# A retention layer and two MLPs in one kernel: which engine prepares the operands of the first span, of the fourth product and of the second layer

## The chip, the cores and the metric

The kernel runs on one core of one Trainium2 chip. TensorE (PE) multiplies, VectorE (DVE), ScalarE (ACT) and GpSimd (POOL) prepare and finish its operands, and SyncE (SP) issues every DMA. The metric is the time of one execution on the device in microseconds; the median of three runs is quoted. Lower is better.

## The reference

```python
gamma = 1.0 - 2.0 ** (-5.0 - np.arange(8))
for t in range(768):                         # retention, batch 4, 8 heads of 64
    state = gamma * state + einsum('bhd,bhe->bhde', k[:, :, t], v[:, :, t])
    y[:, :, t] = einsum('bhd,bhde->bhe', q[:, :, t], state) / 8
x = y.transpose(0, 2, 1, 3).reshape(3072, 512)
h = x @ w_in;  x = (h * cos(h)) @ w_out      # layer 1, 512 -> 2048 -> 512
h = x @ w_in2                                # layer 2, the same sizes
g = where(h >= 1, h, where(h <= -1, 0, (h + 1) ** 2 / 4))
return g @ w_out2
```

All arrays are float32.

## The kernel before

**Retention.** The 768 steps are cut into 6 chunks of 128, and the heads into 4 pairs, which gives 24 units. A unit has four input tiles of 128x512: q and k by columns, k and v by rows. q is multiplied by a table of decays (`scale_q`), k by rows by another (`scale_k`). PE makes `scores(u)` from k and q; DVE writes them, masked, to SBUF (`mask`); PE makes `outputs(u)` from v, the masked scores and the state of its head pair; PE makes `outer(u)`, which is added to the state (`update_state`).

**The two layers.** Each layer's first product, x times the up weights, is done with seven products p1 to p7 of half size instead of eight (a Strassen form), so that sums of quarters of x and of the weights are needed: s3, s2 and s1 are the sums behind p7, p6 and p5, and a fourth, s4 = x12 - s2, is the operand of p3. Every operand goes to PE as a pair of reduced-precision parts: ACT copies the number to the high part (`split_high` to `x_hi`, `t_high` to `tw`, `wd_high` to `wd_hi`, `gate_high` to `g_hi`), and then the low part is the number minus the high part (`split_low` and `gate_low` on DVE, `t_low` and `wd_low` on POOL). A product is then three matmuls for each of two contraction tiles, so six in all, of 128x512 output (L489, L491, L493); a down product (`down`, L518 to L524) is twelve.

**The order.** There are six spans, each of 2 chunks (1024 rows): three for layer 1 and three for layer 2. A span has 8 quads. Quad q > 0 is p1, p6, a down product, p2, p7, p5, a down product, p4, p3. After the quads a tail of 18 down products runs; in it, between the down products, the units of the next span are worked (spans 1 and 2), or the x of the next span comes back from DRAM (`x2_scratch`) and is summed and split (before spans 3, 4 and 5). Each engine's order is written out by hand in its own loop, and engines meet only at semaphores: an engine that waits holds back all that is behind it in its loop.

**The prologue** (L530 to L544 on PE, L784 to L794 on DVE, L992 to L1000 on ACT, L1099 to L1113 on POOL) works the 8 units of span 0. DVE scales q of units 0 and 1, POOL scales q of units 2 to 7 and k of all 8, and at unit 4 sums the first quad's up weights (`t_sums(0)`, `t_sums(1)`); `t_low(0)` and `t_low(1)` stand before the q of unit 7 and after it:

```python
for u in range(AHEAD):          # POOL, L1105
    if u >= 2:
        scale_q(u)
    scale_k(u)
    if u == 4:
        t_sums(0)
        t_sums(1)
    if u in (6, 7):
        t_low(u - 6)
```

As the loop shows, `t_low(0)` follows unit 6 and so precedes `scale_q(7)`. PE's p1 and p7 of quad 0 (`EARLY_PRODUCTS`) stand between `outer(6)` and `outputs(7)`. The weights of quad 1 are split by ACT and POOL inside quad 0.

**The queues.** SP's one queue issues every load in the order of the sync block. The up weights of a quad land in one half of a ring of two (`raw`, `tw`); in the spans 0 and 3 (`made(s)`) they are summed and split there and stored to `t_scratch`, in the others they are read back from it. The down weights of a layer are split once. Layer 1's are split one pair per quad of span 0 (`wd_high(0, q)`, `wd_low(0, q)`). Layer 2's are split in the tail of span 2 for q = 0 to 5 (L1029, L1136) and in the first two quads of span 3 for q = 6 and 7 (L976, L1124). The sums of x for layer 2 are eight POOL instructions per span (`x2_sum_s3`, `x2_sums_rest`, L1079); those of layer 1 are eight DVE instructions per span (`x_sum`: L643, and L629 for s4), and all fourteen low parts of x are DVE's (L653 from PSUM, L656 from SBUF).

Of the kernel before, what the change touches and what calls it, by code (L numbers as in the profile page):

```python
# [7 lines left out]
F32 = mybir.dt.float32  # L8
# [32 lines left out]
EARLY_PRODUCTS, LATER_PRODUCTS = ["p1", "p7"], ["p2", "p6", "p5", "p4", "p3"]  # L41
# [9 lines left out]
SPLITS = [("p1", 0, X11), ("p1", 1, X11 + 1), ("p2", 0, X12), ("p2", 1, X12 + 1), ("p7", 0, X11), ("p7", 1, X11 + 1),  # L51
          ("p4", 0, X22), ("p6", 0, SUM2), ("p5", 0, X21), ("p3", 0, X12),
          ("p4", 1, X22 + 1), ("p6", 1, SUM2 + 1), ("p5", 1, X21 + 1), ("p3", 1, X12 + 1)]
NS = len(SPLITS)
SUMS_BEFORE = {4: 1, 5: 2, 7: 3, 8: 4, 9: 5, 11: 6, 12: 7, 13: 8}
NSUM = 8
# [17 lines left out]
SPLITS_LATE = [[0], [1], [2], [3], [4], [5], [6], [7], [8, 9], [10, 11], [12, 13], []]  # L74

SPLITS_OF = [[0], [1], [2], [3], [4], [5], [6, 7, 8, 9], [10, 11, 12, 13]]
# [15 lines left out]
def retention_mlp_kernel(nc, q_t, k_t, k_n, v_n, w1u, w1d, w2u, w2d, table, out):  # L92
# [7 lines left out]
    with ExitStack() as ctx:  # L100
# [17 lines left out]
        tb = sb("tb", [P, TABLE_WIDTH])  # L118
        half_one = sb("half_one", [P, 1])
        probe = sb("probe", [P, 1])  # L120

# [12 lines left out]
        kn_sb = nc.alloc_sbuf_tensor_at("kn_sb", [P, N], F32, offset=place + 8 * N * 4)  # L134

# [74 lines left out]
        q_scaled_first, q_scaled, kn_scaled = sem("q_scaled_first"), sem("q_scaled"), sem("kn_scaled")  # L210
        scores_done, masked = sem("scores_done"), sem("masked")
        y_done, outer_done, state_done = sem("y_done"), sem("outer_done"), sem("state_done")
        x_copied = sem("x_copied")
        x2_summed = sem("x2_summed")
        x2_in = [sem(f"x2_in{i}") for i in range(8)]
        summed, xhi_done, xlo_done = sem("summed"), sem("xhi_done"), sem("xlo_done")
        raw_in = [[sem(f"raw_in{i}_{kt}") for kt in range(2)] for i in range(2)]
# [153 lines left out]
        def _(pe):  # L371
            def y_taken(u):
# [3 lines left out]
                if i < KT:  # L376
                    pe.wait_ge(xlo_done, NS * s + i + 1)
                elif i < COPIES:
                    pe.wait_ge(summed, NSUM * s + i - KT + 1)
                else:  # L380
                    pe.wait_ge(xlo_done, NS * s + (7 if i == COPIES else 11))
                    pe.wait_ge(summed, NSUM * s + (4 if i == COPIES else 7))

# [23 lines left out]
            def outputs(u):  # L407
# [12 lines left out]
                if has_state:  # L420
                    pe.wait_ge(state_done, 2 * (u - KT + 1))
# [12 lines left out]
            def outer(u):  # L434
# [3 lines left out]
                pe.wait_ge(kn_scaled, u + 1)  # L438
                if u < AHEAD:
                    if u >= 2:  # L440
# [731 lines left out]
```

## Time and profile before

| what | value |
|---|---|
| median of 3 runs | 1144.98 us |
| lowest, highest | 1143.63, 1147.88 us |
| the profiled execution: its time | 1146.63 us |
| the profiled execution: its span | 1144.8 us |
| PE busy in the span | 1104.1 us, 96% |
| DVE, ACT, POOL busy | 709.8, 506.3, 261.6 us |

The span is what the profiler saw from the first to the last instruction; the execution's own time is 1.8 us more. Busy time of PE counts overlapping matmuls, so a busy share near 1 does not say at which pace they start: the number of matmuls in a stretch does. The page names a line of the kernel for every group, and the tile that is written before the arrow, the tiles that are read behind it.

### The profile page before, as it was taken

How to read it: one execution, taken by the hardware profiler on the slowest of the kernel's cores; microseconds unless marked ns; L12 is line 12 of the kernel's file. 1: busy time of each engine (PE TensorE's matmuls, PEld its weight loads, DVE VectorE, ACT ScalarE, POOL GpSimd, SP SyncE). 2: the span in 40 equal slices, each digit the busy share in tenths (PEclk: the TensorE clock that was granted, in tenths of full speed). 3: DMA queues.
4: the chain of work that ended last, by engine and by line, in shares of the span. 5: the costliest groups of instructions: out<-in, count | busy, mean ns of one | idle time of the engine just before them, and what ended most of it. 6: DMA issues, size and time to landing. Idle time of an engine off the chain costs nothing.

```text
span 1144.8 us, 14409 instructions
## 1 busy us (share of the span) xinstructions
PE 1104.1 (96%) x5572; PEld 893.7 (78%) x5572; DVE 709.8 (62%) x1016; ACT 506.3 (44%) x822; POOL 261.6 (23%) x251
## 2 busy tenths in 40 slices
PE   7789999989999999999997999999999999999998
PEld 6667777877888787788875788887888887888887
DVE  5677775474666646466659677656566647566642
ACT  2367764234656423565654343434322334333232
POOL 6366652320000120000118565504000004000000
PEclk8899999999999999999999999999999999999999
DMA  9234553442333243233233633343233331233111
GB/s 342 102 121 183 202 208 124 148 138 110 129 129 126 105 139 120 101 129 129 83 104 118 237 116 141 159 171 133 101 129 129 116 114 74 102 129 129 65 38 37
DMA packets 44452, 149.12 MB, mean 130 GB/s; under 512 B 4704, under 2 KB 4832, under 8 KB 42336
## 3 DMA queue, kind: packets, MB, share of 16 engines
q1 hardware_dynamic: 44384, 148.20, 36.1%
q8 instruction: 44, 0.72, 0.3%
q14 instruction: 24, 0.20, 0.1%
HBM read 106.24 MB, written 41.94 MB: 129 GB/s over the span
## 4 chain that ended last, share of the span: by engine, by line
PE 69%; DVE 12%; ACT 8%; POOL 3%; DMA 3%; issue 3%; SPq 1%; DVEq 0%; ACTq 0%
PE bank L489 11%; PE bank L493 10%; PE bank L491 10%; PE bank L522 7%; PE bank L524 7%; PE bank L523 7%; PE bank L518 5%; PE bank L519 4%; PE bank L520 4%; DVE g_lo L714 4%; ACT work L927 2%; DVE x_lo L656 2%; ACT work L929 2%; PE bank L402 2%; DMA kn_sb<-in_k_n 2%
## 5 line engine op out<-in xcount | busy, mean ns | idle before, releaser
L489 PE MATMUL bank<-x_hi,tw 128*128 128x512 f32 x672 | 269.0, 400 | 9.7 <-ACT work L900 4.1
L491 PE MATMUL bank<-x_lo,tw 128*128 128x512 f32 x672 | 266.9, 397 | 0.0
L493 PE MATMUL bank<-x_hi,tw 128*128 128x512 f32 x672 | 266.8, 397 | 0.0
L518 PE MATMUL bank<-g_hi,wd_hi 128*128 128x512 f32 x384 | 154.2, 402 | 11.7 <-DVE g_lo L714 10.9
L489 PEld LDWEIGHTS bank<-x_hi,tw 128*128 128x128 f32 x672 | 127.5, 190 | 44.8 <-DVE late L705 4.0
L493 PEld LDWEIGHTS bank<-x_hi,tw 128*128 128x128 f32 x672 | 127.6, 190 | 30.3
L522 PE MATMUL bank<-wd_hi,g_hi 128*128 128x512 f32 x384 | 150.3, 391 | 0.8 <-DVE g_lo L714 0.8
L519 PE MATMUL bank<-g_lo,wd_hi 128*128 128x512 f32 x384 | 150.7, 392 | 0.0
L520 PE MATMUL bank<-g_hi,wd_lo 128*128 128x512 f32 x384 | 150.5, 392 | 0.0
L491 PEld LDWEIGHTS bank<-x_lo,tw 128*128 128x128 f32 x672 | 127.7, 190 | 29.1
L524 PE MATMUL bank<-wd_hi,g_lo 128*128 128x512 f32 x384 | 149.8, 390 | 0.0
L523 PE MATMUL bank<-wd_lo,g_hi 128*128 128x512 f32 x384 | 149.6, 389 | 0.0
L714 DVE SCALAR_TENSOR_TENSOR g_lo<-late,g_hi 128x512 fp32r<-128x512 f32 x96 | 85.2, 887 | 90.0 <-ACT g_hi L943 89.6
L943 ACT ACTIVATE g_hi<-late 128x512 fp32r<-128x512 f32 x96 | 60.3, 630 | 151.0 <-PE bank L520 80.5
L714 DVE SCALAR_TENSOR_TENSOR g_lo<-work,g_hi 128x512 fp32r<-128x512 f32 x96 | 85.7, 892 | 42.6 <-ACT g_hi L943 40.6
L931 ACT ACTIVATE work<-work,half_one 128x512 f32<-128x512 f32 x96 | 66.9, 720 | 94.3 <-DVE work L694 94.3
L943 ACT ACTIVATE g_hi<-work 128x512 fp32r<-128x512 f32 x96 | 60.7, 632 | 92.3 <-DVE work L708 54.7
L518 PEld LDWEIGHTS bank<-g_hi,wd_hi 128*128 128x128 f32 x384 | 72.4, 188 | 34.5 <-DVE g_lo L714 17.0
L1079 POOL TENSOR_TENSOR work<-work 128x512 f32<-128x512 f32 x24 | 37.4, 1586 | 219.1 <-DVE x_lo L656 219.1
L522 PEld LDWEIGHTS bank<-wd_hi,g_hi 128*128 128x128 f32 x384 | 72.1, 188 | 18.0 <-DVE g_lo L714 2.9
L520 PEld LDWEIGHTS bank<-g_hi,wd_lo 128*128 128x128 f32 x384 | 72.5, 189 | 15.9
L524 PEld LDWEIGHTS bank<-wd_hi,g_lo 128*128 128x128 f32 x384 | 72.1, 188 | 15.4
(91 smaller groups left out, 1467.8 us busy)
## 6 DMA issues: line engine op xcount, KB each, us to landing
tw<-t_scratch SPq DMA_DIRECT2D x64, 896.0 KB, 6.3
t_scratch<-tw SPq DMA_DIRECT2D x16, 1792.0 KB, 7.8
work<-x_scratch SPq DMA_DIRECT2D x24, 256.0 KB, 3.7
raw<-in_w1u SPq DMA_DIRECT2D x16, 256.0 KB, 3.1
wd_raw<-in_w1d SPq DMA_DIRECT2D x8, 512.0 KB, 8.9
q_sb<-in_q_t SPq DMA_DIRECT2D x16, 256.0 KB, 2.9
k_sb<-in_k_t SPq DMA_DIRECT2D x16, 256.0 KB, 3.8
v_sb<-in_v_n SPq DMA_DIRECT2D x16, 256.0 KB, 4.1
```

The lines of the kernel that those rows point to most:

```text
L489: nc.tensor.matmul(to[:, :], w[:, kt, 0, i, :], x_hi[:, i, kt, :], start=opens, stop=False, skip_group_check=True)
L491: nc.tensor.matmul(to[:, :], w[:, kt, 0, i, :], x_lo[:, i, kt, :], start=False, stop=False, skip_group_check=True)
L493: last = nc.tensor.matmul(to[:, :], w[:, kt, 1, i, :], x_hi[:, i, kt, :], start=False, stop=kt == 1, skip_group_check=True)
L518: nc.tensor.matmul(to[i][:, :], wd_hi[:, f, cols], g_hi[:, slot, :], start=opens, stop=False)
L519: nc.tensor.matmul(to[i][:, :], wd_hi[:, f, cols], g_lo[:, slot, :], start=False, stop=False)
L520: last = nc.tensor.matmul(to[i][:, :], wd_lo[:, f, cols], g_hi[:, slot, :], start=False, stop=closes)
L522: nc.tensor.matmul(to[i][:, :], g_hi[:, slot, cols], wd_hi[:, f, :], start=opens, stop=False)
L523: nc.tensor.matmul(to[i][:, :], g_hi[:, slot, cols], wd_lo[:, f, :], start=False, stop=False)
L524: last = nc.tensor.matmul(to[i][:, :], g_lo[:, slot, cols], wd_hi[:, f, :], start=False, stop=closes)
L714: nc.vector.scalar_tensor_tensor(out=g_lo[:, d % 2, :], in0=g, scalar=2.0 if s < PAIRS else 1.0, in1=g_hi[:, d % 2, :].bitcast(F32), op0=A ...
L931: nc.scalar.activation(t, t, ACT.Square, scale=0.5, bias=half_one[:, 0:1]).then_inc(square_done, 1)
L943: nc.scalar.activation(g_hi[:, d % 2, :], g, ACT.Copy, scale=2.0 if s < PAIRS else 1.0).then_inc(ghi_done, 1)
```

## The change

**Prologue.** The k of the first 8 units is scaled by ACT (`scale_k` there, two instructions of 256 columns per unit) and no longer by POOL. The first state of each head pair (units 0 to 3) is copied from PSUM by ACT (`copy_state`) and not by DVE. POOL does q of units 2 to 5, the sums of quad 0's weights, q of 6 and 7, then the low parts of quad 0's weights, the sums and low parts of quad 1's, whose high parts ACT does in the prologue too. PE's p1 and p7 move behind the last unit, and quad 0's order is p1, p7, p2, p6, p5, p4, p3. DVE masks two units ahead.

**The operand of p3.** In spans 0, 1 and 2 the sum s4 and its low part move from DVE to POOL (`x3_operand`), four instructions per span; the high part stays with ACT, at the end of its list. In all spans `sum_u3` and `sum_h22` of quad 0 now wait for these low parts.

**Layer 2.** The eight sums of x per span move from POOL to DVE (`x2_sum`), and the high and low parts stand in another order, spread over the tail (`SUMS_LATE`, `HIGHS_LATE`, `LOWS_LATE`). All eight pairs of the second layer's down weights are split within the quads of span 3.

**Addresses.** The tables `tb`, `half_one` and `probe` (656 + 1 + 1 columns) are allocated behind the weight ring and no longer ahead of it, so the ring lies lower in each partition.

```diff
-EARLY_PRODUCTS, LATER_PRODUCTS = ["p1", "p7"], ["p2", "p6", "p5", "p4", "p3"]
+FIRST_OF_ALL = ["p1", "p7", "p2", "p6", "p5", "p4", "p3"]
+SUMS_LATE = {3: [("s3", 0), ("s3", 1)], 4: [("s2", 0), ("s1", 0)], 5: [("s4", 0)], 6: [("s2", 1), ("s1", 1)], 7: [("s4", 1)]}
+HIGHS_LATE = {0: [("p1", 0), ("p1", 1)], 1: [("p2", 0), ("p2", 1)], 4: [("p7", 0), ("p7", 1)], 5: [("p4", 0), ("p6", 0)],
+              6: [("p5", 0), ("p3", 0)], 7: [("p4", 1), ("p6", 1)], 8: [("p5", 1), ("p3", 1)]}
+LOWS_LATE = {1: [("p1", 0), ("p1", 1)], 2: [("p2", 0), ("p2", 1)], 4: [("p7", 0)], 5: [("p7", 1), ("p4", 0)], 6: [("p6", 0)],
+             7: [("p5", 0), ("p3", 0)], 8: [("p6", 1)], 9: [("p5", 1), ("p4", 1), ("p3", 1)]}
@@ PE
-            for u in range(AHEAD):
+            for u in range(AHEAD - 2):
                 outputs(u)
-                if u + 2 < AHEAD:
-                    scores(u + 2)
+                scores(u + 2)
                 outer(u)
-                if u == AHEAD - 2:
-                    pe.wait_ge(masked, 2 * (AHEAD - 1))
-                    for name in EARLY_PRODUCTS:
-                        product(0, 0, name)
+            outputs(AHEAD - 2)
+            outputs(AHEAD - 1)
+            outer(AHEAD - 2)
+            outer(AHEAD - 1)
@@ DVE
             def operands(s, i, lows=()):
...
+                    x_sum(s, "s2", kt)
+                    x_sum(s, "s1", kt)
+                    if s == 0:
+                        update_state(AHEAD - 2)
+                    split_low(s, "p6", kt)
+                    if lows:
+                        gate_low(s - 1, *lows.pop(0))
+                    split_low(s, "p5", kt)
+                    split_low(s, "p4", kt)
+                    for item in lows:
+                        gate_low(s - 1, *item)
@@ sum_u3, and in the same way sum_h22 with 2 * (s + 1)
                 if q == 0:
                     dve.wait_ge(u2_done, n + 1)
+                    dve.wait_ge(x3lo_done, 2 * s + 1)
@@ DVE, prologue
+            scale_q(1)
             mask(0)
-            scale_q(1)
-            dve.wait_ge(zeroed, KT)
+            mask(1)
             for u in range(AHEAD):
-                if u + 1 < AHEAD:
-                    mask(u + 1)
-                update_state(u)
                 operands(0, u)
+                if u + 2 < AHEAD:
+                    mask(u + 2)
+                if KT <= u < AHEAD - 2:
+                    update_state(u)
+            update_state(AHEAD - 1)
@@ DVE, tail before a span of layer 2
-                        if s + 1 < SPANS and n:
-                            for m in SPLITS_LATE[n - 1]:
-                                split_low(s + 1, m)
+                        if s + 1 < SPANS:
+                            for which, kt in SUMS_LATE.get(n, []):
+                                x2_sum(s + 1, which, kt)
+                            for name, kt in LOWS_LATE.get(n, []):
+                                split_low(s + 1, name, kt)
@@ ACT
-                if s == PAIRS and q in (0, 1):
-                    wd_high(1, QUADS - 2 + q)
-                more = n < QUADS * SPANS and made(n // QUADS)
+                more = 1 < n < QUADS * SPANS and made(n // QUADS)
...
-                if s == 0:
-                    wd_high(0, q)
+                if made(s):
+                    wd_high(s // PAIRS, q)
...
+            for u in range(3):
+                scale_k(u)
             for u in range(AHEAD):
                 operands(0, u)
-                if u == 4:
-                    t_high(0)
-                    t_high(1)
-                if u == AHEAD - 2:
-                    copy_p1(0, 0)
+                if u + 3 < AHEAD:
+                    scale_k(u + 3)
+                if u < KT:
+                    copy_state(u)
+                if u in (3, 4, 5):
+                    t_high(u - 3)
+                if u == 6:
+                    t_high(3)
@@ POOL
+            def x3_operand(s, kt):
+                x = work[:, X12 + kt, :]
+                pool.wait_ge(x_copied, COPIES * s + 2 + kt + 1)
+                pool.wait_ge(summed, NSUM * s + SUM_PLACE["s2", kt] + 1)
+                nc.gpsimd.tensor_tensor(x, x, work[:, SUM2 + kt, :], ALU.subtract).then_inc(x3_summed, 1)
+                pool.wait_ge(x3hi_done, 2 * s + kt + 1)
+                nc.gpsimd.tensor_tensor(x_lo[:, BLOCK["p3"], kt, :], x, x_hi[:, BLOCK["p3"], kt, :].bitcast(F32),
+                                        ALU.subtract).then_inc(x3lo_done, 1)
...
+            for u in range(2, 6):
+                scale_q(u)
+            t_sums(0)
+            t_sums(1)
+            scale_q(6)
+            scale_q(7)
+            t_low(0)
+            t_low(1)
+            t_sums(2)
+            t_sums(3)
+            t_low(2)
+            t_low(3)
+            x3_operand(0, 0)
+            x3_operand(0, 1)
             for s in range(SPANS):
                 for q in range(QUADS):
...
-                    if s == 0:
-                        wd_low(0, q)
-                    if s == PAIRS and q in (0, 1):
-                        wd_low(1, QUADS - 2 + q)
+                    if made(s):
+                        wd_low(s // PAIRS, q)
                 if s < PAIRS - 1:
...
+                    x3_operand(s + 1, 0)
+                    x3_operand(s + 1, 1)
```

## Rows read from the trace of the kernel before

**Rows 1.** The page, part 1: PE's line of the span.

```profile
PE 1104.1 (96%) x5572; PEld 893.7 (78%) x5572; DVE 709.8 (62%) x1016; ACT 506.3 (44%) x822; POOL 261.6 (23%) x251
```

**Rows 2.** Windows: stretch, length, busy time and count of each engine, granted clock, DMA.

```profile
40.00:60.00 20.00, 16.99 (x122) 13.57 (x119) 16.46 (x28) 8.23 (x14) 6.04 (x10) 0.81 0.33 119
60.00:80.00 20.00, 16.33 (x62) 12.24 (x62) 14.43 (x17) 13.27 (x22) 12.01 (x12) 0.91 0.42 145
...
603.00:640.40 37.40, 31.19 (x125) 23.82 (x125) 33.80 (x22) 16.15 (x25) 28.94 (x14) 0.95 0.26 85
...
80.00:184.00 104.00, 101.70 (x433) 80.48 (x431) 75.91 (x102) 74.31 (x119) 62.32 (x60) 1.00 0.54 191
...
300.00:380.00 80.00, 80.00 (x348) 65.23 (x347) 51.88 (x79) 47.77 (x79) 0.00 (x0) 1.00 0.31 115
660.00:760.00 100.00, 100.00 (x435) 81.48 (x434) 70.19 (x101) 41.40 (x60) 47.80 (x53) 1.00 0.41 155
780.00:800.00 20.00, 19.61 (x85) 15.42 (x84) 15.12 (x15) 8.76 (x16) 11.02 (x7) 1.00 0.17 67
```

**Rows 3.** Timeline of PE: start, length, line, tiles, count, idle before and its releaser.

```profile
24.93 1.16 PE L402 MATMUL bank<-first_in 64*128 64x128 f32 x16 [1.43 <-POOL first_in L1040]
...
37.20 2.00 PE L402 MATMUL bank<-late 64*128 64x128 f32 x16 [4.55 <-POOL late L1040]
...
43.00 0.50 PE L489 MATMUL bank<-x_hi,tw 128*128 128x512 f32 x1
...
45.89 1.05 PE L425 MATMUL bank<-late,state 128*128 128x128 f32 x8
...
47.80 0.64 PE L446 MATMUL bank<-late 128*64 128x64 f32 x16
...
63.44 0.50 PE L489 MATMUL bank<-x_hi,tw 128*128 128x512 f32 x1 [1.12 <-POOL tw L1068]
...
71.34 0.71 PE L489 MATMUL bank<-x_hi,tw 128*128 128x512 f32 x1 [2.08 <-ACT work L900]
...
255.96 0.50 PE L518 MATMUL bank<-g_hi,wd_hi 128*128 128x512 f32 x1 [1.12 <-DVE g_lo L714]
```

**Rows 4.** Timeline of POOL in the prologue and in quad 0.

```profile
23.52 1.27 POOL L1040 TENSOR_TENSOR first_in<-first_in,tb 128x512 f32<-128x512 f32 x1
...
35.79 1.26 POOL L1040 TENSOR_TENSOR late<-late,tb 128x512 f32<-128x512 f32 x1
...
61.28 2.10 POOL L1068 TENSOR_TENSOR tw<-raw,tw 128x896 fp32r<-128x896 f32 x1 [2.53 <-ACT tw L877]
```

**Rows 5.** The load of the last q: its issue on SP's queue, and its microseconds to landing.

```profile
16.93 0.36 SPq L247 DMA_DIRECT2D late<-in_q_t  x1
...
late<-in_q_t SPq DMA_DIRECT2D x1, 256.0 KB, 10.0
```

**Rows 6.** Timelines of DVE and of POOL in the tail of span 2.

```profile
602.53 0.68 DVE L656 TENSOR_TENSOR x_lo<-work,x_hi 128x512 fp32r<-128x512 f32 x1
...
606.23 1.78 DVE L656 TENSOR_TENSOR x_lo<-work,x_hi 128x512 fp32r<-128x512 f32 x1
...
622.01 2.88 DVE L656 TENSOR_TENSOR x_lo<-work,x_hi 128x512 fp32r<-128x512 f32 x1
...
603.21 12.74 POOL L1079 TENSOR_TENSOR work<-work 128x512 f32<-128x512 f32 x8 [25.20 <-DVE x_lo L656]
615.92 11.19 POOL L1075 TENSOR_TENSOR wd_lo<-wd_raw,wd_hi 128x1024 fp32r<-128x1024 f32 x4
```

**Rows 7.** Groups by line and shape: count, then busy time and mean ns of one.

```profile
L491 PE MATMUL bank<-x_lo,tw 128*128 128x512 f32 x672 | 266.9, 397 | 0.0
L519 PE MATMUL bank<-g_lo,wd_hi 128*128 128x512 f32 x384 | 150.7, 392 | 0.0
...
L877 ACT ACTIVATE tw<-raw 128x896 fp32r<-128x896 f32 x32 | 29.9, 939 | 1.5 <-POOL raw L1063 1.5
...
L1051 POOL TENSOR_TENSOR late<-late,tb 128x512 f32<-128x512 f32 x4 | 4.2, 1040 | 7.0 <-DMA late<-in_k_n 6.9
```

More of the change, by code:

```diff
@@ L456, in product @@
                 if q == 0:
-                    pe.wait_ge(xlo_done, NS * s + max(m for m in range(NS) if SPLITS[m][0] == name) + 1)
+                    if name == "p3":
+                        pe.wait_ge(x3lo_done, 2 * (s + 1))
+                    else:
+                        pe.wait_ge(xlo_done, NS * s + LOW_PLACE[name, 1] + 1)
                     if name in ("p7", "p4"):
@@ new lines, in split_low @@
+            def split_low(s, name, kt):
+                hi = x_hi[:, BLOCK[name], kt, :].bitcast(F32)
+                lo = x_lo[:, BLOCK[name], kt, :]
+                if name == "p3":
+                    dve.wait_ge(x3hi_done, 2 * s + kt + 1)
+                    nc.vector.tensor_tensor(lo, work[:, X12 + kt, :], hi, ALU.subtract).then_inc(x3lo_done, 1)
+                    return
+                slot = HIGHS[HIGH_PLACE[name, kt]][2]
+                dve.wait_ge(xhi_done, NS * s + HIGH_PLACE[name, kt] + 1)
+                if s < PAIRS and name not in SUM_OF:
+                    if name != "p4":
+                        dve.wait_ge(x_copied, COPIES * s + slot + 1)
+                    nc.vector.scalar_tensor_tensor(out=lo, in0=unit_banks(AHEAD * s + slot)[2][:, :], scalar=SCALE, in1=hi,
+                                                   op0=ALU.mult, op1=ALU.subtract).then_inc(xlo_done, 1)
@@ L840, in copy_x, with split_high @@
                 nc.scalar.activation(work[:, i, :], unit_banks(u)[2][:, :], ACT.Copy, scale=SCALE).then_inc(x_copied, 1)
-            def split_high(s, m):
-                name, kt, slot = SPLITS[m]
-                if s < PAIRS and m not in SUMS_BEFORE:
+            def split_high(s, name, kt):
+                hi = x_hi[:, BLOCK[name], kt, :]
+                if name == "p3":
+                    act.wait_ge(x3_summed, 2 * s + kt + 1)
+                    nc.scalar.activation(hi, work[:, X12 + kt, :], ACT.Copy).then_inc(x3hi_done, 1)
+                    return
+                slot = HIGHS[HIGH_PLACE[name, kt]][2]
+                if s < PAIRS and name not in SUM_OF:
@@ new lines, in scale_k, with copy_state @@
+            def scale_k(u):
+                p = u % KT
+                act.wait_ge(kn_in_first[u], 16)
+                for h in range(2):
+                    part = unit_kn(u)[:, :, h, :]
+                    last = nc.scalar.activation(part, part, ACT.Copy, scale=decay_k[:, 2 * p + h:2 * p + h + 1])
+                last.then_inc(kn_scaled_first, 1)
+            def copy_state(u):
+                act.wait_ge(outer_done, u + 1)
+                act.wait_ge(zeroed, u + 1)
+                for h in range(2):
+                    part = slice(h * DH, (h + 1) * DH)
+                    nc.scalar.activation(state[part, u, :, part],
+                                         unit_banks(u)[3][part, 0:B * DH].rearrange("p (b e) -> p b e", b=B),
+                                         ACT.Copy).then_inc(state_copied, 1)
@@ L1116, in _ @@
                     n = QUADS * s + q + 1
[L1117 removed]
+                    if 1 < n < QUADS * SPANS and made(n // QUADS):
                         t_sums(weight_item(n, 0))
```

237 lines of the change are left out of this document (103 added, 134 removed).

## The prediction, made before the kernel was changed

> **What bounds the kernel now.** I read the shares of the span first [rows 1]: PE is busy for 1104 of 1145 us, so an edit to ACT, DVE or POOL pays only where PE stands still or loses its clock. The windows [rows 2] show where. At its best pace PE starts 348 matmuls in 80 us (4.35 per us, 0.23 us each), in a window where POOL does nothing. Against that pace: 603 to 640.4 has 125, which 28.7 us would hold, so 8.7 us are lost; 80 to 184 has 433 in 104 us, so 4.5 us are lost; 780 to 800 has 85 in 20 us, 0.5 us lost; 660 to 760 loses nothing although POOL is busy for half of it. From 40 to 80 us the granted clock is 0.81 and 0.91, and PE idles for 7 us. The change touches all of these but 300 to 380, so each part is costed where PE stood.
>
> The timelines say why. In the tail of span 2 the same low part on DVE takes 0.68 us alone, 1.78 beside POOL's sums and 2.88 beside POOL's `wd_low` [rows 6]: the two engines take turns, each instruction waiting out the other's. In the prologue PE waits 4.55 us at 37.20 for the q of unit 7, which POOL scales at 35.79, behind `t_low(0)`, although it had landed at 16.93 + 10.0 = 26.9 us [rows 3 to 5]. Quad 1 starts at 63.44, held by `t_low` of its own weights, which POOL begins at 61.28 and which waited for ACT [rows 3, 4].
>
> **Part 1, prologue up to unit 7.** POOL's order is now q5, the sums of quad 0, q6, q7, with no k at all. The wait at 24.93 for q5 (1.43 us) shrinks, since q5 stands ahead of the sums: I take 0.9 of it. q7 no longer waits for `t_low(0)`: landed at 26.9, behind sums and q6, it is scaled at about 29 us, before PE can use it, so the 4.55 us go whole. Scores of unit 7 then start at 37.20 - 4.55 - 0.9 = 31.75. From there PE's own work to the first product is what it was: 5.8 us from 37.20 to 43.00, and 2.55 us for `outputs(7)` and `outer(7)` (45.89 to 47.80 + 0.64 [rows 3]); before `outputs(7)` I add 1 us for its mask, which stands behind s3's two instructions and POOL's turns on DVE. First product: 41 us, with all eight units done; before, this was 50.5.
>
> Who pays for that: ACT has 16 more instructions for k and 8 for the state. No row has this shape on ACT. Above, an instruction of 896 columns takes 0.94 us [rows 7], so 256 columns cost no more; below, nothing. I take 0.4 us each, by its share of the columns plus a fixed part, so 0.8 for a unit's k where POOL took 1.04 [rows 7]. They fall in ACT's gaps between units (ACT waits for PE's outputs), so I cost them at nothing; at 0.94 each, ACT would run 24 x 0.54 = 13 us more, half of it under the loads, and y of the last units would come some 4 us later.
>
> **Part 2, quad 0 and the start of quad 1.** p1, p7, p2, p6, p5 run from 41 to 48 (five times 6 x 0.23 = 1.4 us). Then p4 needs `sum_u3`, and p3 needs `sum_h22`; both now wait for p3's operand. Its chain starts when POOL has finished quad 1's `t_low(3)`, which I place at 43.1: the high part on ACT stands behind that of p5 for unit 6 and ends at 41.0, and POOL adds 2.1 [rows 4]. From 43.1: sum 1.3 (as a q on POOL [rows 4]), one turn of DVE 0.7, high part 0.6 (512 columns, by the 0.94 of 896 [rows 7]), low part 1.3, second sum 1.3, high part 0.6, low part 1.3, `sum_h22` 0.7: 7.8 us, so p3 can start at 51 and ends at 52.4. The weights of quad 1 have been ready since 43, so quad 1 starts at 52.4 and not 63.44: 11 us gained. Inside quad 1 the first down product needs `wd_low(0, 0)`, which cannot be earlier than its high part (at 53.5, behind quad 0's gate) and 1.1 for that high part and 2.8 on POOL (11.19 / 4 [rows 6]): 57.3, a stall of 2 us where PE had 0.5. But the p2 behind it was held at 71.34 by ACT's copy of p1, and its new date, by the same chain of down product, gates and sums without POOL's turns, is 60.3: still 11 us. I assume one fall of the clock to 1.2 GHz behind that stall, as there was one at 71.34 (0.71 us for a matmul there, 0.50 at 63.44). **Sum: -11.0 us**, from -14 (no x3 chain on the path) to -5 (ACT at 0.94 us, POOL waiting a turn at every step).
>
> **Part 3, spans 1 and 2.** DVE loses four instructions of 0.68 us at each transition, of which three stood ahead of the late `gate_low` that holds PE for 1.12 us at 255.96 [rows 3]. The order is shorter by one instruction there, so I take 0.6 us at this transition and 0.4 at the next. POOL's four instructions fall beside eleven microseconds of down products. **-1.0**, from -2 to +2 (POOL's turns delaying the last gates, or `sum_u3` waiting).
>
> **Part 4, tail of span 2 and the next two.** POOL has nothing left there. DVE has a down product's gate and at most three sums or low parts per down product: 4 x 0.61 = 2.44 us, against 12 x 0.23 = 2.76 us of PE. Each sum's inputs stand one down product or more ahead in the three lists, so that no engine waits in order. SP's order is unchanged, and the x tiles had landed when POOL used them at 603.21 [rows 6], before DVE will. So the whole loss goes: **-8.7** in span 2, **-0.5** in each of the two others, -9.7 in all; from -10.5 to -6.
>
> **Part 5, down weights in the quads of span 3.** Six more `wd_high` and `wd_low` there, one per quad. The model is span 0, which loses 4.5 us in 104 with POOL at 60%; but its DVE and ACT carry the cosine. Layer 2's window of 660 to 760 loses nothing with POOL at 48%, and `wd_low` would bring it to some 60%. I take +0.5, between 0 and +4.5, nearer the second because it is the same gate code.
>
> **Part 6, addresses.** A product's matmul takes 397 ns and a down product's 392 [rows 7], both 128x512. No row shows why. The ring's address may have a part in it or none: bounds 5 ns x 2016 matmuls, 10 us either way; I take 0, because no row ties a duration to a place.
>
> **Sum.** -11.0 - 1.0 - 9.7 + 0.5 = -21.2 us. The profiled execution took 1146.63 us, 1.65 above the median of 1144.98; its span of 1144.8 would become 1123.6 and its time 1125.4. Against the median: **1123.8 us**.
>
> **A rule against the change.** DVE does these two-input instructions in 0.68 us, and POOL takes 1.3 for a tile of the same size [rows 4, 6]: the operand of p3 moves to the slower engine and stands on the path in quad 0. The Trainium skill, "GPSIMD Engine Reference", section 4.1, says the same, that elementwise work with two inputs belongs on VectorE because GpSimd is about twice as slow; with the rows' durations for DVE the four steps would cost 2.4 us less in part 2. The skill's "SBUF — State Buffer", Terms, has the two engines share one pair of ports by a lock held for the whole instruction; the trace agrees by 1.78 and 2.88 against 0.68 us, and no estimate above needs the rule.
>
> **The rivals.**
> 1. *p3's operand takes over the wait in the prologue.* ACT and DVE wait in order for POOL (`turns` of quad 0 stands behind ACT's last high part of p3), so each turn lost on POOL moves everything. For it: POOL's chain has no slack in part 2. Against it: POOL's other work ends at 43. With 7 us more the time is 1131.
> 2. *The second layer's weights cost what the first's do.* +4 us more: 1128. For it: span 0; against it: the calm window of layer 2.
> 3. *The sums on DVE wait for the loads.* If the x tiles land after DVE asks, DVE holds the gates behind it and PE stops as before: half of part 4 comes back, 1128.5. Against it: POOL found them landed.
> 4. *The ring's new place makes product matmuls shorter* by up to 5 ns: 1114.
> 5. *Slower than before: the new place makes them longer.* Every product reads its weights from the ring. It decides from 21.2 us / 2016 = 10.5 ns per matmul on; at 14 ns the time is 1152. For it: the products are the slower kind already. Against it: the difference seen between two places and kinds is 5 ns.
>
> **How the numbers follow.** Forecast 0.66 (its own range 1118 to 1128), rival 1 0.13, rival 2 0.08, rival 3 0.04, rival 4 0.07, rival 5 0.02. The range of 8 in 10 takes in rivals 1 to 3 whole and a part of the fourth: 1116 to 1132. A measurement of this kernel tells 0.5%, 5.7 us, from no change. All cases but the fifth lie below 1139, so faster 0.95; rivals 1 and 3 together could end within it: same 0.03; slower 0.02.
>
> **What would show it.** Right: the first p1 of quad 0 near 41 us, p3 of it near 51, quad 1 near 52 to 53; PE's idle time before `down` on `gate_low` gone between 580 and 660; DVE's low parts of layer 2 at 0.69 us each in the tails and POOL idle there; some 88 matmuls per 20 us in span 3's quads. Wrong: a wait on `x3lo_done` over 3 us, on scores for a k scaled late by ACT, or on `wd_low` in span 3, or another mean for L491 than 397 ns.

## The result, and the profile after

The changed kernel takes **1113.65 us** (median of 4 runs, 1112.70 to 1114.66); the kernel before took 1145.99 in the 4 runs beside it (1143.63 to 1147.88). The ratio is 0.972 [0.970, 0.974]: 32 us less. The forecast was 1123.8, and the range ended at 1116.0, 2.4 us above the result. The profiled execution took 1114.66 us, its span is 1112.9.

The page of the changed kernel, its first line and its shares of the span, as [rows 1]:

```profile
span 1112.9 us, 14425 instructions
PE 1082.4 (97%) x5572; PEld 888.3 (80%) x5572; DVE 682.1 (61%) x1020; ACT 515.9 (46%) x846; POOL 232.9 (21%) x231
```

PE's busy time fell by 21.7 us (from 1104.1) with the same 5572 matmuls. An edit that only took stalls away would leave busy time as it was, unless the clock changed too. So either matmuls ran at a higher clock or something else happened; the next view shows both. (Two kernels below part the 21.7 us: with the ring back in its old place PE's busy time is 1094.4, so 9.7 go with the schedule and 12.0 with the ring.) Windows: the window, its length, busy time with instructions of PE, PE's weight loads, DVE, ACT and POOL, the granted clock, the DMA share and GB/s, as [rows 2]:

```profile
40.00:60.00 20.00, 17.31 (x79) 12.71 (x75) 16.22 (x24) 11.49 (x20) 13.55 (x14) 1.00 0.40 142
60.00:80.00 20.00, 18.18 (x78) 14.31 (x78) 13.31 (x20) 14.86 (x24) 11.30 (x13) 1.00 0.47 174
290.00:360.00 70.00, 70.00 (x311) 57.95 (x310) 46.39 (x71) 42.38 (x71) 0.00 (x0) 1.00 0.36 132
570.00:616.00 46.00, 45.61 (x201) 37.45 (x201) 25.06 (x40) 19.85 (x35) 0.00 (x0) 1.00 0.46 149
620.00:640.00 20.00, 17.86 (x71) 14.07 (x70) 16.32 (x21) 10.52 (x15) 17.29 (x21) 0.91 0.67 271
640.00:740.00 100.00, 100.00 (x442) 82.78 (x442) 71.38 (x101) 45.65 (x65) 61.48 (x58) 1.00 0.43 159
```

Three things stand here. The tail of span 2 (570 to 616) is full: 201 matmuls in 46 us, 4.37 per us, where [rows 2] have 125 in 37.4. The clock is at full speed from 40 to 80 us, where it was 0.81 and 0.91. And the calm window of 290 to 360 has 4.44 per us, *more than the 4.35 that the prediction called PE's best pace*. Nothing in the calm stretch waits, before or after. The matmuls themselves start sooner after each other. The lines of the product and of the down product, as [rows 7] (line, matmul, tiles and shape; busy us, mean ns of one; idle before):

```profile
L510 PE MATMUL bank<-x_lo,tw 128*128 128x512 f32 x672 | 262.2, 390 | 0.0
L538 PE MATMUL bank<-g_lo,wd_hi 128*128 128x512 f32 x384 | 150.1, 391 | 0.0
```

The product's matmul was 397 ns and is 390, the down product's was 392 and is 391. These durations overlap, so they give a sign and not a size. The size is the mean time from one matmul's start to the next, worked out from all the trace's matmuls inside a product or a down product: 232.7 ns before and 227.0 after in products, 227.7 and 227.3 in down products. 2016 product matmuls x 5.7 ns = 11.5 us.

**Where the 32 us lie.** I set each span's first product, and each tail's first down product, of one trace against the other's (us):

| stretch | gained |
|---|---|
| start to the tail of span 0 | 12.1 |
| transitions into spans 1 and 2 | -0.7, +0.2 |
| quads of spans 1 and 2 | 1.9, 1.9 |
| transition into span 3 | 9.3 |
| quads of span 3 | 0.4 |
| transitions into spans 4 and 5 | 1.1, 1.1 |
| quads of spans 4 and 5, last tail | 2.3, 2.3, 0.0 |

The quads of a span hold 336 product matmuls, so 5.7 ns each makes 1.9 us: the quads of spans 1 and 2 gain that by the pace alone. Those of spans 4 and 5 gain 2.3, and that is the ring's as well: in `ring_back` below they gain 0.0. The prologue's timeline (start, duration, engine, line, operation, tiles, and in brackets the wait and its releaser), as [rows 3], with one row from span 3 at its end:

```profile
31.59 1.16 PE L417 MATMUL bank<-late 64*128 64x128 f32 x16
37.18 1.13 PE L440 MATMUL bank<-late,state 128*128 128x128 f32 x8 [1.70 <-DVE late L618]
40.19 0.50 PE L508 MATMUL bank<-x_hi,tw 128*128 128x512 f32 x1
50.81 0.47 PE L508 MATMUL bank<-x_hi,tw 128*128 128x512 f32 x1 [0.64 <-DVE work L779]
52.27 0.39 PE L508 MATMUL bank<-x_hi,tw 128*128 128x512 f32 x1
56.41 0.47 PE L537 MATMUL bank<-g_hi,wd_hi 128*128 128x512 f32 x1 [1.26 <-issue]
59.25 0.49 PE L508 MATMUL bank<-x_hi,tw 128*128 128x512 f32 x1
628.39 0.79 PE L508 MATMUL bank<-x_hi,tw 128*128 128x512 f32 x1 [1.47 <-POOL tw L1137]
```

Scores of unit 7 at 31.59 (forecast 31.75), the first product at 40.19 (41), p3 of quad 0 at 50.81 (51), quad 1 at 52.27 (52.4), its first down product at 56.41 (57.3), its p2 at 59.25 (60.3). POOL's line, as [rows 4], shows p3's operand being made; both its low parts stand behind ACT for 0.74 us:

```profile
42.96 1.28 POOL L1151 TENSOR_TENSOR work<-work 128x512 f32<-128x512 f32 x1
44.98 1.57 POOL L1153 TENSOR_TENSOR x_lo<-work,x_hi 128x512 fp32r<-128x512 f32 x1 [0.74 <-ACT x_hi L892]
46.52 1.29 POOL L1151 TENSOR_TENSOR work<-work 128x512 f32<-128x512 f32 x1
48.55 1.29 POOL L1153 TENSOR_TENSOR x_lo<-work,x_hi 128x512 fp32r<-128x512 f32 x1 [0.74 <-ACT x_hi L892]
```

And DVE in the tail of span 2, as [rows 6]: the low part takes 0.69 us where it took up to 2.88 beside POOL.

```profile
592.08 0.69 DVE L753 SCALAR_TENSOR_TENSOR g_lo<-late,g_hi 128x512 fp32r<-128x512 f32 x1 [0.82 <-ACT g_hi L1013]
592.69 1.29 DVE L672 TENSOR_TENSOR work<-work 128x512 f32<-128x512 f32 x2
593.89 0.69 DVE L690 TENSOR_TENSOR x_lo<-work,x_hi 128x512 fp32r<-128x512 f32 x1
```

### The profile page after: what moved, and what is told of

The parts are those of the page before. It is cut to its first block, busy times and chain, and to the rows that moved or that the text cites. A ratio compares the mean times of both kernels' runs of the same rounds, so it can differ in the third digit from the quotient of the medians.

```text
span 1112.9 us, 14425 instructions
## 1 busy us (share of the span) xinstructions
PE 1082.4 (97%) x5572; PEld 888.3 (80%) x5572; DVE 682.1 (61%) x1020; ACT 515.9 (46%) x846; POOL 232.9 (21%) x231
## 4 chain that ended last, share of the span: by engine, by line
PE 74%; ACT 9%; DVE 6%; POOL 4%; DMA 3%; issue 2%; SPq 1%; DVEq 0%; ACTq 0%; POOLq 0%
PE bank L508 10%; PE bank L510 10%; PE bank L512 10%; PE bank L541 8%; PE bank L543 8%; PE bank L542 8%; PE bank L537 6%; PE bank L538 5%; PE bank L539 5%; ACT work L997 2%; ACT work L999 2%; DVE g_lo L753 2%; PE bank L417 2%; DMA kn_sb<-in_k_n 1%; DVE work L723 1%
## 5 line engine op out<-in xcount | busy, mean ns | idle before, releaser
L508 PE MATMUL bank<-x_hi,tw 128*128 128x512 f32 x672 | 264.0, 393 | 8.1 <-DVE late L744 3.9
L510 PE MATMUL bank<-x_lo,tw 128*128 128x512 f32 x672 | 262.2, 390 | 0.0
L512 PE MATMUL bank<-x_hi,tw 128*128 128x512 f32 x672 | 262.0, 390 | 0.0
L537 PE MATMUL bank<-g_hi,wd_hi 128*128 128x512 f32 x384 | 153.4, 400 | 5.4 <-DVE g_lo L753 3.5
L541 PE MATMUL bank<-wd_hi,g_hi 128*128 128x512 f32 x384 | 149.4, 389 | 0.0
L753 DVE SCALAR_TENSOR_TENSOR g_lo<-late,g_hi 128x512 fp32r<-128x512 f32 x96 | 68.8, 717 | 90.8 <-ACT g_hi L1013 90.5
L537 PEld LDWEIGHTS bank<-g_hi,wd_hi 128*128 128x128 f32 x384 | 72.3, 188 | 25.9 <-DVE g_lo L753 7.4
L541 PEld LDWEIGHTS bank<-wd_hi,g_hi 128*128 128x128 f32 x384 | 72.1, 188 | 14.9
L542 PEld LDWEIGHTS bank<-wd_lo,g_hi 128*128 128x128 f32 x384 | 72.1, 188 | 14.9
```

What stands on the lines that cost most here:

```text
L508: nc.tensor.matmul(to[:, :], w[:, kt, 0, i, :], x_hi[:, i, kt, :], start=opens, stop=False, skip_group_check=True)
L510: nc.tensor.matmul(to[:, :], w[:, kt, 0, i, :], x_lo[:, i, kt, :], start=False, stop=False, skip_group_check=True)
L512: last = nc.tensor.matmul(to[:, :], w[:, kt, 1, i, :], x_hi[:, i, kt, :], start=False, stop=kt == 1, skip_group_check=True)
L537: nc.tensor.matmul(to[i][:, :], wd_hi[:, f, cols], g_hi[:, slot, :], start=opens, stop=False)
L541: nc.tensor.matmul(to[i][:, :], g_hi[:, slot, cols], wd_hi[:, f, :], start=opens, stop=False)
L542: nc.tensor.matmul(to[i][:, :], g_hi[:, slot, cols], wd_lo[:, f, :], start=False, stop=False)
```

## The experiments

The theory after the result: the schedule brings the 21 us of the forecast, and the ring's new place brings about 10 more. The rival: the schedule brings all of it, and the pace of matmuls is a by-product. Every kernel below was timed in three rounds beside the kernel before, whose medians there were 1146.75, 1146.63 and 1146.2 us.

**Place and schedule apart.** The kernel before with the changed kernel's order of tiles, and the changed kernel with the order of before:

```diff
 state = sb("state", [P, KT, B, P])
-tb = sb("tb", [P, TABLE_WIDTH])
-half_one = sb("half_one", [P, 1])
-probe = sb("probe", [P, 1])
...
 kn_sb = nc.alloc_sbuf_tensor_at("kn_sb", ...)
+tb = sb("tb", [P, TABLE_WIDTH])
+half_one = sb("half_one", [P, 1])
+probe = sb("probe", [P, 1])
```

> The kernel before with one edit, the three tables allocated behind the ring. Theory A (the ring's place sets the pace of the product matmuls): a product matmul starts every 0.227 us as in the changed kernel and not every 0.2326 us, 2016 of them give 11.7 us back, so about 1134 us, all else as before. Rival B (the place is nothing; the pace came with the new schedule, because other engines touch the ring or the x tiles at other times): 1146 us and 0.2326 us.

Measured: 1135.97 us (1135.22 to 1138.84), ratio 0.991 [0.988, 0.994]. Nothing but three lines moved, and 10.8 us are gone; its trace has nearly none of it before the tail of span 0, and 1.7 to 2.5 us from each tail's start to the next.

> The changed kernel with the three tables ahead of the ring again. Theory A: product matmuls at 0.2326 us, about 1125 us, which is where the prediction put the whole change. Rival B: 1113.7 us and 0.227 us.

Measured: 1123.87 us (1122.39 to 1126.68), ratio 0.980 [0.977, 0.982]: the schedule alone is worth 22.9 us, and the ring's place 10.2 on top. The two sides add up within the spread of the runs, so the effects are independent as far as these times can tell.

**Which place?** The tables are 2632 bytes in each partition, so the ring went down by 2688, from 196352 to 193664 after rounding. Before, every other tile that PE reads (`wd_hi` at 1152, `x_hi` at 66688, `g_hi` at 156800) stood 128 bytes above a multiple of 256, and the ring alone, with the retention tiles that share its second half, stood at one. Afterwards all have the same remainder. That leaves two readings: the ring's own address counts, or only how it lies to the operand that streams past it. A gap of 32 columns (128 bytes) ahead of the ring, or ahead of all tiles, tells them apart:

```diff
+gap = sb("gap", [P, 32])        # ring_up_128: ahead of the ring
+gap = sb("gap", [P, 32])        # all_up_128: ahead of wd_hi, the first tile
```

> The changed kernel with 128 unused bytes per partition ahead of the ring. Before the change the ring began at a multiple of 256 bytes, after it at 128 above one, as the x, gate and down-weight tiles do. Theory A1 (it is the ring's place within 256 or 512 bytes): slow products, 0.2326 us, about 1125 us. Theory A2 (it is how high in the partition the ring lies): 128 bytes are nothing, 0.227 us and 1113.7 us.

> The changed kernel with 128 unused bytes per partition ahead of all tiles, so that ring, x, gates and down weights all begin at a multiple of 256 bytes. If what counts is the weights' own place within 256 bytes (A1a): products and down products both at 0.2326 us, 4320 matmuls x 5.8 ns = 25 us, about 1139 us. If it is the ring's place relative to the tile that streams against it (A1b), or height (A2): nothing changes, 1113.7 us.

Measured: 1122.11 us (1120.96 to 1122.39) with the ring alone moved, 1111.55 (1110.52 to 1112.65) with everything moved. The ring begins at the same address, 193792, in both, and one is slow and the other fast: not its own address. Two further kernels test the relation from its other side. One puts the gap ahead of `x_hi`, so that x, g and the ring move together while the down weights stay; the other uses half the gap ahead of the ring.

```diff
+gap = sb("gap", [P, 32])        # x_and_ring_up_128: ahead of x_hi, behind wd_hi and wd_lo
+gap = sb("gap", [P, 16])        # ring_up_64: ahead of the ring, 64 bytes
```

> The changed kernel with 128 unused bytes ahead of the x tiles: x, gates and ring move together, the down weights stay. Theory A1b (a matmul is slower when the weights' tile and the streamed tile begin at different places within 256 bytes): products stay at 0.227 us and the down products fall to about 0.2326 us, 2304 x 5.8 ns = 13 us, so about 1127 us. If the ring's own place within 256 bytes were the cause (products slow, down products untouched): products 0.2326 us, 1125 us. If neither: 1113 us.

> The changed kernel with 64 unused bytes ahead of the ring. If any difference in place within 256 bytes slows a matmul: product matmuls near 0.2326 us, 1122 to 1125 us. If only a half of 256 bytes matters, as tried so far: 0.227 us, 1113.7 us.

Measured: 1125.17 us (1124.24 to 1126.37) and 1123.82 (1122.78 to 1125.27). The lines of the product and of the down product are the verdict here, and the sign flips with the tile that was moved. First the kernel with the ring 128 bytes up, then the one with x, g and ring up:

```profile
L511 PE MATMUL bank<-x_lo,tw 128*128 128x512 f32 x672 | 265.4, 395 | 0.0
L539 PE MATMUL bank<-g_lo,wd_hi 128*128 128x512 f32 x384 | 149.9, 390 | 0.0
```

```profile
L511 PE MATMUL bank<-x_lo,tw 128*128 128x512 f32 x672 | 261.7, 389 | 0.0
L539 PE MATMUL bank<-g_lo,wd_hi 128*128 128x512 f32 x384 | 152.2, 396 | 0.0
```

By the mean time from start to start (ns):

| kernel | x to ring | g to down weights | product | down |
|---|---|---|---|---|
| before | 128 B apart | equal | 232.7 | 227.7 |
| ring_moved_alone | equal | equal | 227.0 | 227.4 |
| after | equal | equal | 227.0 | 227.3 |
| ring_back | 128 B | equal | 232.7 | 227.6 |
| ring_up_128 | 128 B | equal | 232.7 | 227.6 |
| ring_up_64 | 64 B | equal | 233.5 | 228.3 |
| all_up_128 | equal | equal | 226.8 | 227.2 |
| x_and_ring_up_128 | equal | 128 B | 227.9 | 232.9 |

("Equal" is by the remainder of the tiles' addresses modulo 512; the slices inside a tile lie 512 bytes or more apart and are all of the quick kind.) So a matmul of this form starts 5 to 6 ns later where the tile of its weights and the streamed tile don't have the same remainder, whichever of the two was moved and in products and down products alike.

Two things in these traces narrow it further. The roles don't matter: layer 1's down products (L537) load the down weights and stream the gates, layer 2's (L541) load the gates and stream the down weights, and with x, g and ring up they go from 227.9 to 232.6 ns and from 226.7 to 233.2. And DVE, ACT and POOL don't make it: where all three stand still from 0.2 us before an interval to 0.4 us after it, down products take 233.7 ns in that kernel (165 intervals) and 226.8 in the changed one (140), and products 232.9 before and 226.6 after, though over only 25 intervals each. Outside the rule stay differences of about 1 ns: the down products of `ring_up_64` (228.3) and the products of `x_and_ring_up_128` (227.9) have equal tiles and are a little slow, and no run here explains that.

**The second layer's down weights** back to the tail of span 2, all but the last two, to see what part 5 cost:

```diff
@@ ACT (and POOL's wd_low in the same way)
-if made(s):
-    wd_high(s // PAIRS, q)
+if s == 0:
+    wd_high(0, q)
+if s == PAIRS and q in (0, 1):
+    wd_high(1, QUADS - 2 + q)
@@ ACT's tail
+if s == PAIRS - 1 and n % 2 == 1 and n // 2 < QUADS - 2:
+    wd_high(1, n // 2)
```

> The changed kernel with six of the eight pairs of the second layer's down weights split in the tail of span 2 again, as before. Theory (in part 4, POOL and DVE take turns, and the tail lost 8.7 us to POOL's sums and its wd_low together): POOL's sums stay on DVE, POOL's wd_low come back with 2.8 us per turn for DVE's 0.6, and DVE now has 22 more instructions there: loss of 8 us or more, 1122 to 1130 us. Rival (the tail was lost to the sums on POOL alone): 1114 us, or a little less, since the quads of span 3 have less to do.

Measured: 1117.48 us (1116.04 to 1118.90), ratio 0.974 [0.971, 0.977]. Less than I expected: the transition into span 3 (from the tail's first down product to the span's first product) takes 4.9 us more than in the changed kernel, and the quads of span 3 get 1.5 back. About 0.8 of the 1.5 is the clock, which falls at 628 us in the changed kernel's trace and not in this one. Two windows of its tail, and its row in the waits between 555 and 650 (us waited, times, longest), which in the changed kernel is 1.1 us in 2 times:

```profile
580.00:600.00 20.00, 19.57 (x85) 15.56 (x84) 17.10 (x22) 12.62 (x22) 8.66 (x3) 1.00 0.47 158
600.00:620.00 20.00, 17.08 (x73) 13.15 (x72) 14.10 (x13) 7.53 (x12) 10.08 (x4) 1.00 0.22 79
```

```profile
PE bank L537 <- DVE g_lo L753: 4.4, 6, 1.6
```

With POOL at work for half of the window, DVE's low parts hold PE again. PE's waits for them grow by only 3.3 us, so most of the turns cost it nothing; I take it that DVE has less to do between gates than I thought.

**The sums of layer 2** back on POOL, the new order kept:

```diff
@@ DVE's tail
-for which, kt in SUMS_LATE.get(n, []):
-    x2_sum(s + 1, which, kt)
@@ POOL, end of a span
+elif s + 1 < SPANS:
+    for n in sorted(SUMS_LATE):
+        for which, kt in SUMS_LATE[n]:
+            x2_sum(s + 1, which, kt)      # now on gpsimd
```

> The changed kernel with the eight sums of x per span of layer 2 on POOL again, in the new order. Theory: as in the tail of span 3 before, some 0.5 us per tail, 1.5 to 3 us in all with span 2: 1115 to 1117 us. Rival (they are what held the tail of span 2): 5 us or more there.

Measured: 1118.97 us (1118.43 to 1122.43), ratio 0.976 [0.973, 0.979]. That is 2 to 4 us above what I expected, and the rival (5 us or more in the tail of span 2) isn't met either: its trace loses 2.4, 1.7 and 1.7 us in the three tails, 5.8 in all; by the medians 5.3. The window with POOL's sums, where a full one has 88 matmuls:

```profile
580.00:600.00 20.00, 18.25 (x79) 14.45 (x79) 15.92 (x15) 10.04 (x18) 13.31 (x8) 1.00 0.48 154
```

Back alone, the weights cost 4.9 us in this transition and the sums 2.4, 7.3 together, where it gained 9.3. The other 2.0 need both at once on POOL, or belong to the new order of sums and low parts, or to the clock: in the kernel before it fell for 3.4 us in this tail (0.95 in the window from 603 in [rows 2]), and in neither of these two traces did it. No run here tells the three apart.

**The operand of p3** back on DVE, in all of layer 1:

```diff
@@ DVE, operands()
 split_low(s, "p5", kt)
+x3_sum(s, kt)
...
+x3_sum(s, kt)                   # the second x tile: behind the low part of p4
+if s == 0:
+    update_state(AHEAD - 1)     # from behind operands(), where it is taken out
+split_low(s, "p3", 0)
 for item in lows:
     gate_low(s - 1, *item)
+split_low(s, "p3", 1)
@@ POOL
-x3_operand(0, 0)
-x3_operand(0, 1)
```

> The changed kernel with s4 and the low part of p3 on DVE again in spans 0, 1 and 2, at the end of DVE's list for the last unit. Theory of part 2 (POOL's chain for p3's operand stands on the path of quad 0): the chain shortens by 2 to 3 us, but DVE's list grows by four instructions of 0.6 us ahead of the first sum, so between 2 us less and 1 us more there, and 0 to 1 us more in spans 1 and 2: 1112 to 1115 us. Rival (the move to POOL is what brought the gain of the prologue): 1118 us or more.

Measured: 1116.35 us (1114.63 to 1117.71), ratio 0.973 [0.970, 0.977]. I had expected 1112 to 1115 us. The interval takes in the changed kernel's ratio, so the times alone give a lean and no verdict; the trace says what leans. PE waits in the middle of quad 0, and quad 1 starts at 54.70, 2.4 us later than with the operand on POOL:

```profile
51.86 0.47 PE L508 MATMUL bank<-x_hi,tw 128*128 128x512 f32 x1 [2.14 <-DVE work L783]
```

This trace also has a fall of the clock, from 37.4 to 40.8 us, and the first product comes 1.6 us late by it. That isn't what moves quad 1: `ring_up_128` and `wd_in_tail` have a fall of the same length there, and nine kernels with the changed kernel's code up to here, these two among them, start quad 1 between 51.49 and 52.92. DVE's windows tell the difference, first in the changed kernel, then with the operand on DVE:

```profile
42.00:52.00 10.00, 8.57 (x35) 6.00 (x34) 8.22 (x13) 4.76 (x9) 6.36 (x5) 1.00 0.01 2
42.00:52.00 10.00, 7.29 (x31) 5.39 (x31) 9.72 (x16) 3.27 (x6) 0.93 (x1) 1.00 0.00 2
```

DVE is busy for 9.72 of 10 us. One of its new instructions, the first sum of s4, takes 2.60 us at 40.88, beside POOL's `t_low(3)`.

The engine that makes this instruction in half the time makes the stretch longer, because it is the one that has a queue there, and because it still takes turns with POOL.

**The weights of quad 1** back into quad 0, and the operand of p3 first on POOL:

```diff
@@ ACT and POOL in quad 0
-more = 1 < n < QUADS * SPANS and made(n // QUADS)
+more = n < QUADS * SPANS and made(n // QUADS)
@@ POOL, prologue
-t_sums(2)
-t_sums(3)
-t_low(2)
-t_low(3)
 x3_operand(0, 0)
```

> The changed kernel with quad 1's weights prepared inside quad 0 again: ACT's and POOL's four steps for them stand behind the prologue, as before the change, and p3's operand runs on POOL ahead of them. Theory of part 2 (quad 1 could start early because its weights were ready): p3 of quad 0 comes 3 to 5 us sooner, since POOL's chain for it is free, but quad 1 waits for t_low, which ACT's high parts hold behind quad 0's gates: quad 1 near 58 instead of 54 us or later, 1117 to 1122 us. Rival (the weights are not what the prologue gained by, the order of PE is): 1111 to 1114 us.

Measured: 1118.18 us (1117.77 to 1119.59), ratio 0.976 [0.974, 0.978]. The time is as expected and one step of the reason is not: I had p3 of quad 0 start 3 to 5 us sooner, and it starts 2.8 later.

```profile
53.63 0.77 PE L508 MATMUL bank<-x_hi,tw 128*128 128x512 f32 x1 [4.21 <-DVE work L779]
```

ACT's `t_high` of quad 1 now stands ahead of `turns(0)` and waits for POOL's sums of the weights, so the angle, and `sum_h22` behind it, are late. A wait in order on one engine carried a delay to a product that needs nothing of it. Quad 1 starts 4.1 us later, at 56.33, well outside the 51.49 to 52.92 of the nine kernels with the prologue unchanged.

**k back on POOL**, interleaved with q:

```diff
@@ POOL
+scale_k(0)
+scale_k(1)
 for u in range(2, 6):
     scale_q(u)
+    scale_k(u)
 t_sums(0)
 t_sums(1)
-scale_q(6)
-scale_q(7)
+for u in (6, 7):
+    scale_q(u)
+    scale_k(u)
```

> The changed kernel with the k of the first 8 units on POOL again, two k before the first q and then q and k in turn. POOL then has 8 x 1.04 us more ahead of its chain. Theory (POOL's list sets the prologue): scores of units 2 to 5 are little touched, since the loads set those; q of 7, the low parts of the weights and p3's operand come 2 to 6 us later: 1115 to 1120 us. Rival (ACT's list sets it, with its 24 new instructions): 1113 us or less.

Measured: 1116.89 us (1115.05 to 1118.03), ratio 0.974 [0.972, 0.977]. The first product starts at 41.61, 1.4 us later, and quad 1 at 55.06, 2.8 later, again outside the 51.49 to 52.92. In the changed kernel PE waited behind the first product, up to p3, only for DVE's sums (0.68 and 0.64 us). Here these two waits stay (0.68 and 0.66), and one for ACT's copy of p1 and one of 0.30 for a low part of DVE come ahead of them:

```profile
45.73 0.47 PE L508 MATMUL bank<-x_hi,tw 128*128 128x512 f32 x1 [1.10 <-ACT work L962]
```

**The loads of span 3's first quads.** The changed kernel still loses time at 626 to 630: PE waits for `t_low` of the weights (the 628.39 row above), and the granted clock of the window is 0.91. SP issues the load of quad 1's up weights behind all eight loads of down weights; one kernel moves it ahead of the last six:

```diff
@@ SP
 if s == PAIRS - 1:
+    load_weights(QUADS * PAIRS + 1)
     for q in range(2, QUADS):
         load_wd(1, q)
```

> The changed kernel with one move in SP's queue: the up weights of span 3's quad 1 are loaded ahead of six of the second layer's down weights, whose loads wait for the tail's last down product. In the changed kernel PE waits 0.67 + 1.47 us for t_low near 626 us, and the granted clock falls to 0.91 in that window. Theory: the wait and the fall go, 3 to 4.5 us, about 1110 us. Rival (POOL's work, not the load, is late: ACT or POOL hold it elsewhere): 1113 to 1114 us.

Measured: 1111.30 us (1109.22 to 1112.00), ratio 0.969 [0.967, 0.972]. The same window in its trace, against 71 matmuls at 0.91 above:

```profile
620.00:640.00 20.00, 19.44 (x83) 14.88 (x82) 16.94 (x21) 10.36 (x14) 15.66 (x14) 1.00 0.56 223
```

12 matmuls more in the window, 2.7 us at 0.227 each. The same window of `p3_on_dve`, whose code is the changed kernel's here, has the wait (2.4 us) and no fall of the clock:

```profile
620.00:640.00 20.00, 17.38 (x75) 13.47 (x74) 15.39 (x20) 10.01 (x15) 16.33 (x20) 1.00 0.71 284
```

So 4 of the 12 matmuls are the clock's, and 8, or 1.8 us, are the wait's, which the move of the load took away in both cases. The gain is less than the 3 to 4.5 us that I expected. This kernel and all_up_128 are the quickest measured here; both medians lie 2 us below the changed kernel's, and the intervals of the ratios overlap its own, so neither is shown to be quicker by the times alone.

## Why the prediction was wrong, and where it was right

**The step that failed is part 6.** It said of the ring's address "I take 0, because no row ties a duration to a place" and gave bounds of 10 us either way. The two kernels that move only the tables measure 10.8 and 10.2 us, the upper bound itself. The prediction's own sign of being wrong, another mean for the product's matmul than 397 ns, came: 390. Rival 4 named the mechanism and its time (1114), but had a chance of 0.07, and the range stopped at 1116, inside the bound that the same text had worked out.

The rows of before held more evidence than I used. A product's and a down product's matmul have one shape, one type and one engine, and differ by 5 ns per instruction [rows 7] over thousands of instances; something in the tiles had to differ. The best pace, 4.35 per us, was taken from quads that were themselves slow. "No row ties it to a place" excused me from asking what else could: of the edits, the new address was the one that touched an operand that every product reads and no down product does.

**The rest of the sum was right in total, and partly by luck.** With the ring back the time is 1123.87 us against a forecast of 1123.8, but the kernel before was slower in those rounds, so the gain is 22.9 us and not 21.2. By the dates of the changed kernel's trace the parts came to 12.1, -0.5, 11.5 and -1.9 us gained, where I had 11.0, 1.0, 9.7 and -0.5. Both sum to 21.2 only because errors of 1 to 2 us of either sign cancel.

**Part 1 held.** The wait for the q of unit 7 went whole, and the scores came within 0.2 us. The wait for the mask ahead of `outputs(7)` was 1.70 us where I took 1, and PE's own work there was shorter, since the clock didn't fall. The 50.5 that I set against the first product's 41 is another product's date: p2, with p1 and p7 done. The first product of before started at 43.00, so it came 2.8 us sooner, and with all eight units done instead of seven. ACT's k takes 0.50 us per instruction where I took 0.4 (share of columns plus a fixed part), and the copy of the state 0.37:

```profile
L935 ACT ACTIVATE first_in<-first_in,tb 128x256 f32<-128x256 f32 x8 | 3.6, 500 | 2.7 <-DMA first_in<-in_k_n 2.6
L943 ACT ACTIVATE state<-bank 64x256 f32<-64x256 f32 x8 | 3.0, 369 | 0.1
```

**Part 2 held in its dates and erred in its subtraction.** Every date of quad 0 and 1 was within 1.1 us. But 63.44 in [rows 3] is not the start of quad 1: it is the second half of its p1, held for the low part of the second contraction tile; the quad starts at 61.45. The gain at its p2 was 12.1 us instead of 11.0. The fall of the clock that I assumed behind the stall didn't come: the granted clock is 1.00 from 40 to 80 us. That POOL's slower operand is on the path of p3 was right (0.64 us of wait at 50.81); rival 1 didn't happen, because POOL was free to start it at 42.96.

**The rule against the change was outweighed.** The Trainium skill, "GPSIMD Engine Reference", section 4.1, puts elementwise work of two inputs on VectorE, because GpSimd is about twice as slow. The rows bear this out (1.28 us on POOL, 0.69 on DVE), and yet with DVE doing this operand quad 1 starts 2.4 us later. The rule speaks of an instruction's duration, and the stretch was set by DVE's queue.

**Part 3 gave nothing in this trace:** 0.5 us lost where I took 1.0 gained. In the transition into span 1 PE waits for a load of k, and the matmuls behind it run at a lower clock (the row of the timeline, and then the window around it):

```profile
193.97 1.33 PE L417 MATMUL bank<-q_sb,k_sb 64*128 64x128 f32 x16 [1.94 <-DMA k_sb<-in_k_t]
```

```profile
180.00:200.00 20.00, 18.07 (x160) 15.07 (x157) 8.89 (x15) 3.54 (x7) 3.36 (x3) 0.91 0.36 119
```

That is this execution's: ten other traces with the same code in the transitions into spans 1 and 2 show no fall of the clock there, and gain 0.5 to 2.9 us over the kernel before in the two together. The forecast of 1.0 lies among them.

**Part 4 was 11.5 us, forecast 9.7:** 9.3 in span 2 (8.7) and 1.1 in each of the other two (0.5 each). The fall of the clock in the tail of span 2 of before went too and is part of the 9.3. Rival 3 didn't happen: none of DVE's sums waits for a load in this tail.

**Part 5 was 1.9 us in this trace, forecast 0.5.** The quads of span 3 gained 0.4 us where the others of layer 2 gained 2.3. Rival 2 would have cost 4 more. The late load isn't in the 1.9, since the kernel before waits there as well (PE's row in the waits from 640 to 700; the changed kernel's is 2.1 us in 2 times):

```profile
PE bank L489 <- POOL tw L1068: 1.9, 2, 1.5
```

About 0.8 is the fall of the clock at 628: two kernels with the same code in span 3 and no fall, `p3_on_dve` and `all_up_128`, take 117.7 and 117.6 us for its quads, the changed kernel 118.5. That leaves about 1 us for the splitting itself, and `wd_in_tail`, which splits as before and shows no fall, takes 117.0, so 0.6 less than those two. The forecast of 0.5 was near, then. From 640 to 740 PE has 442 matmuls in 100 us with POOL at 61%, as calm as any window.

## What to carry to other kernels

Measure the time from one matmul's start to the next for each group of the same shape, and not only its waits: a group that is slower by 2% on a full engine is worth more than most stalls, and here the cure was to give the weights' tile and the streamed tile the same remainder of 512 bytes. Where a part's bounds come out as wide as half the forecast gain, the range must hold them, whatever value is taken in the middle. When work is spread over engines, ask which engine has a queue at that moment, not which does the instruction quickest; and read what stands ahead of a load on its queue as closely as what stands ahead of an instruction.

## What the runs showed of the hardware

The effect of the relative place was not expected. For this form (128x512, weights loaded anew for each matmul, PE full) the mean time from start to start is 227 ns where the weights' tile and the streamed tile lie at the same remainder, and 232.7 to 233.5 ns where they are 128 or 64 bytes apart. It holds in both roles: the down products slow down alike where the down weights are loaded (layer 1, 232.6 ns) and where they are streamed (layer 2, 233.2), and it holds where DVE, ACT and POOL stand still (233.7 against 226.8 ns). A difference of a multiple of 512 bytes is harmless; 256 wasn't tried, nor smaller steps than 64. Why it is so stays open: the runs show that it depends on the two tiles together, and nothing of what happens inside. Whether the two tiles meet at a port, in a bank or at the start of the weight load can't be told from these traces.
